# From the seventh attention pair on, TensorE takes two attention steps at a time

## The reference, cut to what matters

```python
scores = q @ k.T / sqrt(64)                 # 4 batches, 8 heads, 576 positions, head size 64
attn = softmax(where(block_i >= block_j, scores, -1e9))   # blocks of 64 positions
x = heads_joined(attn @ v)                  # 2304 tokens x 512
h = x @ moe_w_in                            # 512 -> 2048
x = maximum(0.01 * h, h) @ moe_w_out        # 2048 -> 512
...                                         # per token: skip score, choice of one of 8 experts, two matmuls
```

## Time and profile before

| | before |
|---|---|
| median of three runs | 786.22 us (785.88 to 787.06) |
| profiled execution | 787.97 us, span of the trace 786.2 us |
| busy share of the span: TensorE, VectorE, ScalarE, GpSimd | 97%, 47%, 38%, 19% |
| share of TensorE in the chain that ended last | 91% |
| instructions in the trace | 13538 |

### The profile page before, as it was taken

One profiled execution on the slowest core, in us unless ns is written; L12 is line 12 of the kernel. 1 busy time (PEld: TensorE's weight loads), 2 busy tenths in 40 slices (PEclk: granted clock), 3 DMA queues, 4 the chain that ended last, 5 costly groups with the idle time before them and its releaser, 6 DMA issues.

```text
span 786.2 us, 13538 instructions
## 1 busy us (share of the span) xinstructions
PE 761.7 (97%) x4738; PEld 643.4 (82%) x4738; DVE 368.5 (47%) x771; ACT 301.4 (38%) x711; POOL 148.8 (19%) x193
## 2 busy tenths in 40 slices
PE   7999989999999998999999999999999999999997
PEld 3555878888888887999987877878778879999996
DVE  5667455543343554013355554555554342444644
ACT  4566655544444554234432222222221131333533
POOL 3226564221121231100020000000000031222222
PEclk9999999999999999999999999999999999999999
DMA  4344767554444541365665656556462038777750
GB/s 125 96 126 142 211 197 201 160 143 130 118 137 128 147 116 57 93 214 162 191 174 177 196 150 190 144 178 189 142 192 68 28 114 246 234 226 236 235 172 4
DMA packets 97671, 121.68 MB, mean 155 GB/s; under 512 B 14226, under 2 KB 60578, under 8 KB 97608
## 3 DMA queue, kind: packets, MB, share of 16 engines
q1 hardware_dynamic: 94776, 116.50, 50.4%
q0 software_dynamic: 2080, 3.77, 1.5%
q10 hardware_dynamic: 752, 0.59, 0.2%
HBM read 89.35 MB, written 31.57 MB: 154 GB/s over the span
## 4 chain that ended last, share of the span: by engine, by line
PE 91%; ACT 2%; issue 2%; SPq 1%; DVE 1%; DMA 1%; POOL 1%; DVEq 0%; POOLq 0%; ACTq 0%
PE ps_hid L1731 10%; PE ps_h L1520 9%; PE ps_x L1573 9%; PE ps_x L1575 8%; PE ps_x L1574 8%; PE ps_h L1522 8%; PE ps_h L1521 8%; PE ps_o L1502 5%; PE ps_t L1476 4%; PE ps_y L1743 3%; PE ps_y L1744 3%; PE ps_y L1742 3%; PE ps_s L1427 2%; PE ps_s L1463 2%; PE ps_s L1464 1%
## 5 line engine op out<-in xcount | busy, mean ns | idle before, releaser
L1520 PE MATMUL ps_h<-xh,win_h 128*128 128x384 f32 x384 | 136.5, 355 | 3.1 <-ACT act L977 2.4
L1522 PE MATMUL ps_h<-xh,win_l 128*128 128x384 f32 x384 | 128.9, 336 | 0.0
L1521 PE MATMUL ps_h<-xl,win_h 128*128 128x384 f32 x384 | 128.8, 335 | 0.0
L1573 PE MATMUL ps_x<-wout_h,g_hi 128*128 128x512 f32 x288 | 117.0, 406 | 0.0
L1575 PE MATMUL ps_x<-wout_h,g_lo 128*128 128x512 f32 x288 | 112.5, 391 | 0.0
L1574 PE MATMUL ps_x<-wout_l,g_hi 128*128 128x512 f32 x288 | 112.2, 390 | 0.0
L977 ACT ACTIVATE act<-ps_h 128x384 f32<-128x384 f32 x96 | 47.1, 491 | 154.9 <-PE ps_h L1522 154.9
L965 ACT ACTIVATE prob<-ps_s,neg_max 128x128 f32<-128x128 f32 (+3 forms) x144 | 78.6, 549 | 28.2 <-DVE neg_max L1126 27.6
L1132 DVE COPY pt<-ps_t 128x384 f32<-128x384 f32 (+4 forms) x113 | 48.4, 436 | 82.4 <-PE ps_t L1476 82.1
L1166 DVE TENSOR_TENSOR g_lo<-g_raw,g_hi 128x512 fp32r<-128x512 f32 x72 | 49.5, 688 | 78.0 <-ACT g_hi L987 77.9
L1126 DVE TENSOR_REDUCE neg_max<-ps_s 128x1 f32<-128x128 f32 (+3 forms) x144 | 71.8, 504 | 30.4 <-PE ps_s L1430 15.3
(11 more groups left out here) (185 smaller groups left out, 1053.0 us busy)
## 6 DMA issues: line engine op xcount, KB each, us to landing
w_sb<-in_w SPq DMA_DIRECT2D x64, 512.0 KB, 5.4
hidden<-act SPq DMA_DIRECT2D x96, 192.0 KB, 2.3
g_raw<-hidden SPq DMA_DIRECT2D x72, 256.0 KB, 4.1
k_raw<-in_k_t SPq DMA_DIRECT2D x40, 144.0 KB, 3.1
x2rows<-x SPq DMA_DIRECT2D x18, 256.0 KB, 2.3
out<-x SPq DMA_DIRECT2D x18, 256.0 KB, 2.6
w_stage<-in_w_in SPq DMA_DIRECT2D x16, 256.0 KB, 3.4
w_stage<-in_w_out SPq DMA_DIRECT2D x16, 256.0 KB, 2.8
```

What stands on the lines that cost most here:

```text
L1520: e.matmul(dst, win_h[:, f, kc, :], xh[slot][:, kc, :], start=kc == 0, stop=False)
L1521: e.matmul(dst, win_h[:, f, kc, :], xl[slot][:, kc, :], start=False, stop=False)
L1522: last = e.matmul(dst, win_l[:, f, kc, :], xh[slot][:, kc, :], start=False, stop=kc == KC - 1)
L1573: e.matmul(dst, hi, wout_h[:, f, :], start=f == 0, stop=False)
```

## The change

From step 54 on TensorE's loop goes two steps at a time: the scores of units s + 2 and s + 3, then the first half of the groups of both steps (rounded down: of one group none, of two groups one), then the transposes of units s - 2 and s - 1, then the products with v of both steps, then the other groups. Groups are no longer cut in two: `FILL` gives whole groups, and the part of a group's two steps that was the first is now the step of the whole. The programs of the other engines are not edited, but they read `filled_at`, so they follow where a group now ends.

```diff
 def filled_at(s):
-    return [g for g, part in FILL.get(s, ()) if part]
+    return FILL.get(s, ())
...
-            if g < FC:
-                s = 50 + 34 * n // (2 * FC)
+        if g < FC:
+            s = 50 + 34 * g // FC
...
-                for g, part in FILL[s]:
-                    hidden(g, part)
+                for g in FILL[s]:
+                    hidden(g)
+
+            for s in range(ROW_UNITS, STEPS, 2):
+                for u in (s + 2, s + 3):
+                    if u < N_UNITS:
+                        scores(u)
+                groups = FILL[s] + FILL[s + 1]
+                for g in groups[:len(groups) // 2]:
+                    hidden(g)
+                for u in (s - 2, s - 1):
+                    if u < N_UNITS:
+                        transposes(u)
+                products_with_v(s)
+                products_with_v(s + 1)
+                for g in groups[len(groups) // 2:]:
+                    hidden(g)
```

More of the change, by code:

```diff
@@ L101, in fill_steps @@
     for g in range(N_ATT_HID):
-        for part in range(2):
-            n = 2 * g + part
-            if g < FC:
-                s = 50 + 34 * n // (2 * FC)
[L106 to L112, removed]
+        if g < FC:
+            s = 50 + 34 * g // FC
+        elif g < 3 * FC:
+            s = 86 + 34 * (g - FC) // (2 * FC)
+        elif g < TWO_BANKS:
+            s = 122 + 22 * (g - 3 * FC) // (TWO_BANKS - 3 * FC)
+        else:
+            s = N_UNITS + 5 + g - TWO_BANKS
+        at[s].append(g)
     return at
 def filled_at(s):
-    return [g for g, part in FILL.get(s, ()) if part]
+    return FILL.get(s, ())
 def t_index(u):
@@ L1511, in turn_inverse, with hidden @@
                 e.transpose(ps_o[0:UNITS, B_COLS:B_COLS + P], inv[:, :], ident[:, :]).then_inc(s_invp, 1)
-            def hidden(g, part):
+            def hidden(g):
                 m, f = divmod(g, FC)
@@ L1516, in hidden @@
                 dst = ps_hidden(g)
-                if part == 0:
-                    hidden_waits(g)
-                for kc in range(KC // 2 * part, KC // 2 * (part + 1)):
+                hidden_waits(g)
+                for kc in range(KC):
                     e.matmul(dst, win_h[:, f, kc, :], xh[slot][:, kc, :], start=kc == 0, stop=False)
@@ L1522, in hidden @@
                     last = e.matmul(dst, win_l[:, f, kc, :], xh[slot][:, kc, :], start=False, stop=kc == KC - 1)
-                if part:
-                    last.then_inc(s_h, 1)
+                last.then_inc(s_h, 1)
             def hidden_waits(g):
@@ L1539, in hidden_waits, with products_with_v @@
                     e.wait_ge(s_act, g)
[L1541 to L1546, removed]
+            def products_with_v(s):
                 p, i = divmod(s, UNITS)
@@ L1551, in _ @@
                     turn_inverse(p - 1)
+            scores_of_both(0)
+            for s in range(ROW_UNITS):
+                if ROW_UNITS <= s + 2:
+                    scores(s + 2)
+                if s >= 2:
+                    transposes(s - 2)
+                products_with_v(s)
+                p, i = divmod(s, UNITS)
                 if i in GROUP_AT:
```

## The result

| | before | after |
|---|---|---|
| median of six runs | 786.90 us (785.88 to 787.30) | 818.17 us (817.39 to 821.00) |
| ratio of after to before, 95% interval | | 1.0403 (1.0386 to 1.0419) |
| span of the trace | 786.2 us | 816.3 us |
| TensorE busy, and idle in the span | 761.7, 24.5 us | 770.2, 46.1 us |

The kernel is 4.0% slower, 31.3 us by the medians. The forecast was 811 us, in a range of 793 to 822.

A forecast was written before the change was run, and what follows sets the result against it. TensorE, busy 761.7 of 786.2 us, was taken to bound the kernel. New waits of 33.8 us less savings of 6.8 and 1.5 gave 25 us more: 813 profiled, 811 as the median, range 793 to 822.

The forecast's parts named there:

- the single groups at even steps: At 12 double steps the group's copy delays exponentials that the next scores need: 17.4 us of new waits.
- groups at odd steps: At 11 double steps second scores at positions 4 to 7 wait for an exponential behind the group's copy: 8.9 us.
- the groups' waits for their shared bank: Groups share one bank and wait for its copy, in two places behind copies of transposed tiles: 4.4 us of new waits.
- the clock: Rival: some 35 more waits let the clock fall to 1.2 GHz in places, 47 us more, 858 us; chance 0.02.
- three signs of being wrong: Scores' waits under 10 us; slower with the waits somewhere else (k by DMA, VectorE's copies); or the granted clock falls.
- the prediction's third small term: A score's first matmul after a wait takes 0.1 us more than in a stream, some 25 times: 2.5 us.
- likeliest case: Scores wait behind groups for copy and exponential, with TensorE slower throughout attention: 811 us, 800 to 819; chance 0.75.
- The savings: Old TensorE waits removed, 6.8 us, and fewer changes between kinds of work, 1.5 us (bounds 0 to 3).
- the larger estimate beside it: By the Trainium skill's page, 38 fewer changes of work, if each were a break, save 6 us: a sum of 806 us.
- The other side: Rival: exponentials come early enough behind groups, so only the savings remain: 778 us; chance 0.09.
- Half of it: Rival: the single groups at even steps don't delay the scores: 794 us; chance 0.07.
- The further wait for k: Rival: five position-4 scores ask up to one step earlier for k loaded by DMA: 822 us; chance 0.07.

The follow-up runs named there:

- kernel 6: Changed kernel, but ScalarE copies a group that ends a double step only behind unit s + 2's exponential, a first-half group's copy staying ahead of unit s + 1's: 789.08 us.
- experiment 3: Changed kernel, but a single group of a double step is done in the first half, between scores and transposes, not at the end: 820.27 us, 1.042.

## Why the prediction was right

**The mechanism and its places** were as forecast. 24.2 us of scores' waits in 26 places stand against "some 26 us in more than 20". Read one by one from the timeline, the single groups at even steps make 15.0 us of idle time in 16 places (forecast 17.4), groups at odd steps 7.3 in 8 places (8.9 in 11; the three of 0.25 at position 5 did not show), double step 82 makes 1.5 (0.6), and one place that was not forecast 0.3. The view's idle time starts at the modelled end of the matmul before; from start to start the place of 192.28 lost 1.46 less the 0.24 that such a score takes, 1.2 us, where the forecast had 1.19 and the view says 1.06.

**Term sized too high:** the groups' waits for their shared bank, 4.4 us in 14 places forecast, measured at 1.8 us in 4.

**Terms sized too low or at zero:** k for position 4 was taken as covered; one wait of 0.6 us stayed. And the clock, which stood in the prediction as a rival of chance 0.02, did fall to 1.2 GHz in three stretches. That it might fall is one of the prediction's own three signs of being wrong, so by its own words it was wrong there: its sum puts the clock at nothing. In the stretch shown, the products lost 1.0 us, the seven transposes 0.3 and the first two group matmuls behind them another 0.3 (0.79 against the 0.44 of the earlier trace rows); at that rate three such make some 5 us (an estimate from these rows). The mean granted clock says the same: 0.8% of the span of 816.3 us against 0.2% of 786.2, 5 us more. The rival as stated there, 47 us, did not come; but as a follow-up of the waits the clock belongs into the sum.

The other 3.5 of the 8.5 us by which TensorE's busy time grew can be the waits themselves, by an estimate: a matmul counts as busy to its modelled end, some 0.16 us past the point at which the next would have started (1.22 lost against 1.06 in the view), and the first matmul of a score behind a wait takes 0.11 us longer (94.52 to 94.75 against 192.28 to 192.40; the prediction's third small term). The view lists 43 waits in place of 27; 16 more of them make some 4 us.

**Where the time lies in the range.** 818 is near the top of the 800 to 819 that the prediction gave for its likeliest case. The room above 811 was left for VectorE's late copies, some 8 us; those made one wait of 0.9 us, and the clock filled the room instead. That the time still lay within is in this part luck.

**The savings** were overestimated if anything: kernel 6, with about as many microseconds of waits as the kernel before, still does not get below it, so no gain from fewer changes of work can be seen, neither the 1.5 us of the sum nor the larger estimate beside it. One fall of the clock in kernel 6 could hide a microsecond or two.

**What the rivals came to.** "The other side" fell at once. "Half of it" fell: the single groups did delay. The further wait for k did not come; those waits became shorter. In the changed kernel the chain of the earlier trace rows is what was forecast. As a general rule, that a score waits for the copy of a group, it was too narrow: experiment 3 took the groups away from the scores, and the waits stayed with other members, VectorE's copies and casts. The ring of four banks lets a score look three or four units back; two scores at once, directly behind the work that the follow-up engines have in front, leave no step in between. The two kinds of work tried in that place, groups and transposes, cost about as much as each other: 24.2 and 23.6 us of waits.

## What to carry to other kernels

Before steps of a software pipeline are merged, walk from each wait of the merged block to its releaser in the queue of the other engine: what stands ahead of it there, and when does TensorE issue that? ScalarE's busy share of 38% said nothing about it here, and moving the item that is seen to delay may only bring the next one to the fore. Where such a wait is found, the order on the follow-up engine is one cure: putting copies that nobody waits for soon behind the exponentials that somebody does took 16.7 us off the changed kernel, and 29 in kernel 6. Not merging the steps gave back more, and on single steps with whole groups the same cure made the fastest kernel here.

## What the runs showed of the hardware

The granted clock fell although no wait of TensorE from step 54 on was longer than 1.7 us. In the stretch 92 to 96 us of the changed kernel TensorE waited for 1.25 and 0.84 us and was busy for 1.91 of 4 us, and in the next 4 us the clock was granted at 0.61 on the mean. The other two falls came behind waits of 1.68 us (113.02) and of 1.14 and 0.23 us (283.27 and 283.94). The same pair, 1.14 and 0.23 us, at 329.16 and 329.83 was followed by no fall, so such waits do not always bring one. Kernel 3, with 23.6 us of such waits, was granted 0.50 to 0.57 in four stretches of 4 us:

```profile
88.00:92.00 4.00, 3.95 (x16) 3.98 (x17) 0.00 (x0) 0.75 (x3) 1.27 (x1) 0.57 0.77 236
143.00:147.00 4.00, 4.00 (x18) 3.47 (x19) 1.20 (x2) 0.38 (x1) 0.00 (x0) 0.57 0.29 76
160.00:164.00 4.00, 2.21 (x13) 1.33 (x12) 2.21 (x6) 2.08 (x6) 0.29 (x1) 0.51 0.39 114
164.00:168.00 4.00, 4.00 (x17) 2.49 (x19) 2.14 (x5) 1.62 (x5) 1.12 (x1) 0.50 0.26 68
```

The page of the changed kernel still shows nines for the clock in all 40 slices; only shorter stretches show it. The Trainium skill ("TensorE: Matmul & The Clock Gate", "A second HAM failure mode: psum-queue depth-cycling") names small idle times between groups of matmuls as a way to make the clock swing between its levels; the trace agrees that the clock falls without one long pause, with three such stretches in the changed kernel and none within the work of the one before. The page's idle times are those of another kernel; here they are waits of up to 1.7 us.
